# Fused attention and two expert layers: first k and q split on ScalarE and VectorE, idle products ahead of the scores, and the expert embeddings prepared in the first pair

## The reference

```python
# attention: B, H, S, D = 4, 8, 576, 64
scores = q @ k.T / sqrt(D) + cum[:, None] - cum[None, :]   # cum = cumsum(log(clip(f, 1e-4, 1)))
scores = where(causal, -1e9, scores)
x = softmax(scores) @ v                                    # laid out as 2304 tokens of 512
# dense layer: 512 -> 2048 -> 512
h = x @ w_in
g = where(h >= 1, h, where(h <= -1, 0, (h + 1) ** 2 / 4))
x = g @ w_out
# experts: N, D, E, F = 2304, 512, 8, 1024
xn = x / (norm(x) + 1e-6)
en = expert_emb / (norm(expert_emb) + 1e-6)
logits = xn @ en.T / tau
e = argmax(logits)
out = softmax(logits)[e] * (relu(x @ w1[e]) @ w2[e])
```

## Time and profile before

| | |
|---|---|
| three timed runs | 880.87, 882.09, 882.01 us, median 882.01 |
| the profiled execution | 880.4 us |
| its span, first to last instruction | 878.4 us |
| PE busy | 842.3 us, 96% |
| PEld busy | 796.7 us, 91% |
| DVE busy | 410.5 us, 47% |
| ACT busy | 394.8 us, 45% |
| POOL busy | 366.4 us, 42% |
| share of the chain of waits | PE 88%, ACT 5%, DVE 4%, POOL 1%, issue 1% |
| mean granted TensorE clock | 0.999 |

### The profile page before, as it was taken

The page is one execution under the profiler, slowest core; times in us unless marked ns, Lnnn a source line. Parts: engine busy times, 40 slices in busy tenths (PEclk is TensorE's granted clock), DMA queues, the critical chain, the costliest instruction groups (busy, mean ns, idle before and its releaser), DMA issues.

```text
span 878.4 us, 13981 instructions
## 1 busy us (share of the span) xinstructions
PE 842.3 (96%) x5138; PEld 796.7 (91%) x5139; DVE 410.5 (47%) x1001; ACT 394.8 (45%) x906; POOL 366.4 (42%) x370
## 2 busy tenths in 40 slices
PE   4999999999989999999999999999999999999995
PEld 3888888888989999999999999999998998998984
DVE  3777788886555544444444445454425210210201
ACT  4777777776566534434534444343331211211211
POOL 7755787784465411201201020074411492010394
PEclk9999999999999999999999999999999999999999
DMA  5667888872200121031021021432233364213140
GB/s 181 178 205 219 237 256 256 257 251 80 56 1 1 47 80 49 7 102 52 28 99 54 28 100 50 124 132 61 61 109 96 103 172 132 77 44 120 35 138 25
DMA packets 66334, 94.58 MB, mean 108 GB/s; under 512 B 6662, under 2 KB 42502, under 8 KB 66256
## 3 DMA queue, kind: packets, MB, share of 16 engines
q1 hardware_dynamic: 58160, 79.43, 30.0%
q10 hardware_dynamic: 6336, 9.44, 3.0%
q0 software_dynamic: 1760, 4.72, 1.4%
HBM read 69.82 MB, written 24.27 MB: 107 GB/s over the span
## 4 chain that ended last, share of the span: by engine, by line
PE 88%; ACT 5%; DVE 4%; issue 1%; POOL 1%; DMA 0%; SPq 0%; ACTq 0%; POOLq 0%; DVEq 0%
PE psum L1370 23%; PE psum L1372 22%; PE psum L1371 22%; PE psum L1304 6%; PE psum L1345 6%; PE psum L1329 4%; DVE ptl L1000 1%; PE psum L1310 1%; ACT pth L792 1%; ACT xo L798 1%; PE psum L1425 1%; DVE g L1029 1%; ACT pr L783 1%; PE psum L1424 1%; PE psum L1314 1%
## 5 line engine op out<-in xcount | busy, mean ns | idle before, releaser
L1370 PE MATMUL psum<-xh,winh 128*128 128x384 f32 x384 | 130.9, 341 | 3.5 <-ACT hpos L829 3.5
L1371 PE MATMUL psum<-xl,winh 128*128 128x384 f32 x384 | 128.4, 334 | 0.0
L1370 PE MATMUL psum<-gh,wouth 128*128 128x384 f32 x384 | 128.4, 334 | 0.0
L1372 PE MATMUL psum<-xh,winl 128*128 128x384 f32 x384 | 128.3, 334 | 0.0
L1372 PE MATMUL psum<-gh,woutl 128*128 128x384 f32 x384 | 128.3, 334 | 0.0
L1371 PE MATMUL psum<-gl,wouth 128*128 128x384 f32 x384 | 128.3, 334 | 0.0
L829 ACT ACTIVATE hpos<-psum,minus 128x384 f32<-128x384 f32 x96 | 55.8, 581 | 149.8 <-DVE hclip L1026 149.5
L1029 DVE TENSOR_TENSOR g<-hpos,hsq 128x384 f32<-128x384 f32 x96 | 63.3, 660 | 112.9 <-ACT hsq L831 112.9
L783 ACT ACTIVATE pr<-pr,mmin 128x64 f32<-128x64 f32 (+2 forms) x144 | 81.7, 568 | 38.3 <-DVE mmin L984 38.3
L622 POOL TENSOR_TENSOR xst<-xst 128x384 f32<-128x384 f32 x24 | 24.3, 1012 | 178.7 <-DMA xst<-rinv_d 178.7
L1142 DVE SCALAR_TENSOR_TENSOR hl<-psum,hh 128x384 fp32r<-128x384 f32 x48 | 26.7, 557 | 141.0 <-ACT hh L860 141.0
(11 more groups left out here) (216 smaller groups left out, 1938.2 us busy)
## 6 DMA issues: line engine op xcount, KB each, us to landing
praw<-moe_w SPq DMA_DIRECT2D x48, 256.0 KB, 2.7
qraw<-q SPq DMA_DIRECT2D x16, 576.0 KB, 5.5
vraw<-vk SPq DMA_DIRECT2D x16, 320.0 KB, 2.9
xh<-yh_d SPq DMA_DIRECT2D x20, 256.0 KB, 4.1
xl<-yl_d SPq DMA_DIRECT2D x20, 256.0 KB, 4.5
kraw<-k SPq DMA_DIRECT2D x16, 288.0 KB, 4.4
c<-cum_d SPq DMA_DIRECT2D x32, 144.0 KB, 4.1
xa_d<-xo SPq DMA_DIRECT2D x16, 288.0 KB, 3.7
```

The costliest lines, as they stand in the source:

```text
L1370: nc.tensor.matmul(psum_at, ah, bh, start=start, stop=False)
L1371: nc.tensor.matmul(psum_at, ah, bl, start=False, stop=False)
L1372: return nc.tensor.matmul(psum_at, al, bh, start=False, stop=stop)
```

## The change

- **First split.** k and q of pair 0 are copied to their high parts by ScalarE, right behind its logarithm, and their low parts are made by VectorE, right behind cum. POOL starts with the mask copies. Its split of pair 1 waits for `q_l`.
- **Idle products.** 22 products of 512 columns of `ident_b` with itself go ahead of the first score on TensorE, into bank `PY`. Nothing reads them.
- **Embeddings.** They are loaded at the start, into a part of `xo`, which is free until pair 0's results. The squared sum lies between VectorE's two subtractions, the square root behind ScalarE's copies, the refinement and scaling at n = -1, the transposes on TensorE at n = 0, and the split at n = 1 and 2. In the refinement a tensor_scalar with two pointer scalars stands in place of two tensor_tensor instructions. `attend_early` waits for `ent_ok`, since both use bank 6.
- **Transfers.** v of pair 0 goes behind the first two c transfers instead of ahead of cum, and k and q of pair 1 go ahead of c of pair 1.
- The wait of `y_high(0)` for the embeddings becomes one for the stores of the attention.

```diff
+    WARM = 22
...
-        scratch = ysq[0:E].rearrange("e m t -> e (m t)")
-        emb, emb_sq, norm_e = scratch[:, 0:DM], scratch[:, DM:2 * DM], scratch[:, 2 * DM:2 * DM + 3]
...
+        emb, emb_sq, norm_e = xo[0:E, 0, 0, 0:DM], xo[0:E, 0, 1, 0:DM], xo[0:E, 1, 0, 0:3]
...
             load_qk(0)
-            load_v(0)
+            sp.dma_start(emb, expert_emb).then_inc(emb_in, 16)
+            sp.dma_start(tau_sb[:], tau.unsqueeze(0).to_broadcast([P, 1])).then_inc(emb_in, 16)
             sp.wait_ge(cum_ok, 1)
             sp.dma_start(cum_d, fc).then_inc(cum_out, 16)
             sp.wait_ge(cum_out, 16)
             load_c(0)
+            load_v(0)
+            load_qk(1)
             load_c(1)
-            load_qk(1)
             load_v(1)
...
-            sp.dma_start(emb, expert_emb).then_inc(emb_in, 16)
-            sp.dma_start(tau_sb[:], tau.unsqueeze(0).to_broadcast([P, 1])).then_inc(emb_in, 16)
...
             def split_qk(p):
                 par = p % 2
                 pool.wait_ge(k_in, 16 * (p + 1))
+                if p == 1:
+                    pool.wait_ge(q_l, 1)
...
 
-            split_qk(0)
             pool.wait_ge(const_step, 4)
...
+            act.wait_ge(k_in, 16)
+            nc.scalar.copy(kh[:, 0, :], kraw[:]).then_inc(k_h, 1)
+            act.wait_ge(q_in, 16)
+            nc.scalar.copy(qh[:, 0], qraw[:]).then_inc(q_h, 1)
+            act.wait_ge(esq_ok, 1)
+            nc.scalar.activation(norm_e[:, 1:2], norm_e[:, 0:1], ACT.Sqrt).then_inc(eroot_ok, 1)
...
+                if n == 1:
+                    act.wait_ge(en_turned, 1)
+                    nc.scalar.copy(ent[:, :, 0:E], psum[:, RB, 0:KD * E].rearrange(
+                        "p (k e) -> p k e", e=E)).then_inc(ent_h, 1)
...
-                    act.wait_ge(emb_in, 32)
+                    for b in range(2):
+                        act.wait_ge(x_out[b], 32 * (PAIRS // 2))
+                        act.wait_ge(r_out[b], 16 * (PAIRS // 2))
...
-                if u == 4:
-                    act.wait_ge(esq_ok, 1)
-                    nc.scalar.activation(norm_e[:, 1:2], norm_e[:, 0:1], ACT.Sqrt).then_inc(eroot_ok, 1)
-                if u == 13:
-                    act.wait_ge(en_turned, 1)
-                    nc.scalar.copy(ent[:, :, 0:E], psum[:, RB, 0:KD * E].rearrange(
-                        "p (k e) -> p k e", e=E)).then_inc(ent_h, 1)
...
+            dve.wait_ge(k_h, 1)
+            nc.vector.tensor_tensor(kl[:, 0, :], kraw[:], kh[:, 0, :].bitcast(F32), ALU.subtract).then_inc(k_l, 1)
+
+
+            dve.wait_ge(emb_in, 32)
+            nc.vector.tensor_tensor_reduce(out=emb_sq, in0=emb, in1=emb, scale=1.0, scalar=0.0, op0=ALU.mult,
+                                           op1=ALU.add, accum_out=norm_e[:, 0:1]).then_inc(esq_ok, 1)
+            dve.wait_ge(q_h, 1)
+            nc.vector.tensor_tensor(ql[:, 0], qraw[:], qh[:, 0].bitcast(F32), ALU.subtract).then_inc(q_l, 1)
...
+                if n == -1:
+                    step(nc.vector.reciprocal(tau_inv[:], tau_sb[:]))
+                    dve.wait_ge(eroot_ok, 1)
+                    step(nc.vector.tensor_scalar_max(norm_e[:, 1:2], norm_e[:, 1:2], 1.0e-30))
+                    step(nc.vector.reciprocal(norm_e[:, 2:3], norm_e[:, 1:2]))
+                    step(nc.vector.tensor_scalar(norm_e[:, 2:3], norm_e[:, 2:3], norm_e[:, 0:1], norm_e[:, 1:2], ALU.mult,
+                                                 ALU.add))
+                    step(nc.vector.tensor_scalar(norm_e[:, 2:3], norm_e[:, 2:3], 0.5, 1.0e-6, ALU.mult, ALU.add))
+                    step(nc.vector.reciprocal(norm_e[:, 1:2], norm_e[:, 2:3]))
+                    nc.vector.tensor_scalar(emb, emb, norm_e[:, 1:2], None, ALU.mult).then_inc(en_ok, 1)
+                if n == 2:
+                    dve.wait_ge(ent_h, 1)
+                    nc.vector.tensor_tensor(ent[:, :, E:2 * E], psum[:, RB, 0:KD * E].rearrange(
+                        "p (k e) -> p k e", e=E), ent[:, :, 0:E].bitcast(F32), ALU.subtract).then_inc(ent_ok, 1)
...
-                if u in (3, 8, 13):
-                    embeddings(u)
...
             pe.wait_ge(const_ok, 2)
+
+            for n in range(WARM):
+                nc.tensor.matmul(psum[:, PY, :].rearrange("p (a b) -> p a b", a=4), ident_b[:],
+                                 ident_b[:].unsqueeze(1).to_broadcast([P, 4, P]), start=True, stop=True)
...
                 pe.wait_ge(pt_l, FILLS * p + 2)
                 pe.wait_ge(vsplit, p + 1)
+                pe.wait_ge(ent_ok, 1)
                 if p >= 1:
                     pe.wait_ge(x_late_b, p)
...
+                if n == 0:
+                    pe.wait_ge(en_ok, 1)
+                    for m in range(KD):
+                        x = nc.tensor.transpose(psum[:, RB, m * E:(m + 1) * E], emb[:, m * P:(m + 1) * P],
+                                                ident[0:E, 0:E])
+                    x.then_inc(en_turned, 1)
...
-                if u == 12:
-                    pe.wait_ge(en_ok, 1)
-                    for m in range(KD):
-                        x = nc.tensor.transpose(psum[:, RB, m * E:(m + 1) * E], emb[:, m * P:(m + 1) * P],
-                                                ident[0:E, 0:E])
-                    x.then_inc(en_turned, 1)
```

More of the change, by code:

```diff
@@ L955, in _, with step, refine_root @@
         def _(dve):
+            steps = [0]
+            def step(x):
+                steps[0] += 1
+                x.then_inc(dve_step, 1)
+                dve.wait_ge(dve_step, steps[0])
+            def refine_root(root, square, t):
+                step(nc.vector.tensor_scalar_max(root, root, 1.0e-30))
+                step(nc.vector.reciprocal(t, root))
+                step(nc.vector.tensor_tensor(t, t, square, ALU.mult))
+                step(nc.vector.tensor_tensor(t, t, root, ALU.add))
+                step(nc.vector.tensor_scalar(t, t, 0.5, 1.0e-6, ALU.mult, ALU.add))
+                step(nc.vector.reciprocal(root, t))
             nc.vector.memset(fz, 0.0)
@@ L1058, in _ @@
                     hidden(H_EARLY.index(n))
-            steps = [0]
-            def step(x):
-                steps[0] += 1
-                x.then_inc(dve_step, 1)
-                dve.wait_ge(dve_step, steps[0])
-            def refine_root(root, square, t):
-                step(nc.vector.tensor_scalar_max(root, root, 1.0e-30))
-                step(nc.vector.reciprocal(t, root))
-                step(nc.vector.tensor_tensor(t, t, square, ALU.mult))
-                step(nc.vector.tensor_tensor(t, t, root, ALU.add))
-                step(nc.vector.tensor_scalar(t, t, 0.5, 1.0e-6, ALU.mult, ALU.add))
-                step(nc.vector.reciprocal(root, t))
+                if n == -1:
[12 more added lines that the diff above has]
+                        "p (k e) -> p k e", e=E), ent[:, :, 0:E].bitcast(F32), ALU.subtract).then_inc(ent_ok, 1)
             def y_low(c, blocks):
@@ L1120, in choose @@
                 chain(nc.vector.tensor_tensor(pick[:, part, :], zc[:, 2], by_expert(mc[:, 1]), ALU.is_equal))
-            def embeddings(u):
-                if u == 3:
-                    dve.wait_ge(emb_in, 32)
-                    nc.vector.tensor_tensor_reduce(out=emb_sq, in0=emb, in1=emb, scale=1.0, scalar=0.0,
-                                                   op0=ALU.mult, op1=ALU.add, accum_out=norm_e[:, 0:1]).then_inc(
-                                                       esq_ok, 1)
-                elif u == 8:
-                    step(nc.vector.reciprocal(tau_inv[:], tau_sb[:]))
-                    dve.wait_ge(eroot_ok, 1)
-                    refine_root(norm_e[:, 1:2], norm_e[:, 0:1], norm_e[:, 2:3])
-                    nc.vector.tensor_scalar(emb, emb, norm_e[:, 1:2], None, ALU.mult).then_inc(en_ok, 1)
-                else:
-                    dve.wait_ge(ent_h, 1)
-                    nc.vector.tensor_tensor(ent[:, :, E:2 * E], psum[:, RB, 0:KD * E].rearrange(
-                        "p (k e) -> p k e", e=E), ent[:, :, 0:E].bitcast(F32), ALU.subtract).then_inc(ent_ok, 1)
             def relu_low(at, f_, high, to):
```

## The result

Four timed runs of the changed kernel took 875.8 to 876.4 us, median 876.1; four of before beside them 880.9 to 882.1, median 881.5. The ratio is 0.9939, 95% interval 0.9927 to 0.9952. A second series, made with the experiments, gave 875.8 against 881.1, ratio 0.9937 (0.9925 to 0.9950). The change saves 5.4 us, 0.6%. The traced execution of after took 876.39 (span 874.2), against 880.4 (878.4) of before: 4.0 less.

What follows compares the result with a forecast made beforehand. TensorE's chain bounds the kernel, with losses at the POOL-bound start, the slow first products and two dense-layer waits. Dense layer 3.9 plus start 1.3 gives 5.2 us off the 881.3 mean: 876.1, own range 873.9 to 879.4, 8-in-10 range 873.9 to 880.3.

Steps and rivals of the forecast that it cites:

- The dense layer, 3.9: Dense layer: taking the square root, small instructions, transposes and last copy out saves 3.9 us; 2.7 to 4.1 possible.
- the second gap: Dense layer, TensorE's 1.95 us wait for hpos before 263.54, behind VectorE's eight small instructions: costs 2.11 us.
- The start, 1.3: First two pairs: last exponential of pair 0 and POOL's ql for pair 1 come earlier, saving 1.3 us; bounds 0 and 2.8.
- the first mask: Pair 0's start: it needs c, whose second transfer lands at 11.6, so it starts at about 11.8 us.
- the last exponential of pair 0: End of pair 0: summed durations put it at 21.45 us against 22.79, 1.3 earlier; called the weakest part.
- v of pair 0 is issued at 9.0 and lands after 3.0: Pair 1's split on POOL: v lands at 12.0, so ql of pair 1 is ready at 20.15, 1.6 us earlier.
- ql of pair 1 later than 21 us: Sign of being wrong about v's landing time; the forecast had ql of pair 1 ready at 20.15 us.
- products of 448 columns at 0.57 after 12 us: Sign on TensorE in the start that its clock is at half rate, against the forecast.
- Clock falls once: Rival, chance 0.08: TensorE's clock falls again before pair 1, losing 3.1 us; total gain 2.1, time 879.2.
- Held steps: Rival, chance 0.22: POOL holds VectorE's embedding tensor_scalar steps in the start, which loses 0.85 us or more; time 879.8.
- More than the sum: Rival, chance 0.08: POOL is not late and the ring keeps its slack; start gives 2.8, total 6.7, time 874.6.
- Slower: Rival, chance 0.06: TensorE stays at 1.2 GHz through pairs 0 and 1, costing 8.6 us against 3.9; time 886.0.

Runs made afterwards that it cites:

- Kernel 10: Before, with the refinement's two one-element tensor_tensor instructions replaced by one tensor_scalar, embeddings still in the dense layer; median 878.2 us, ratio 0.9967.
- kernel 9: Before, with idle products (3 and 8) filling TensorE's two gaps in the dense layer; median 880.6 us, ratio 0.9993.
- Kernel 4: After, with v of pair 0 issued before the wait for cum, k and q of pair 1 behind the first c; median 876.1 us, ratio 0.9935.
- kernel 7: Kernel 4 with the embedding steps ahead of VectorE's first mask and 14 idle products ahead of pair 1; median 875.0 us, ratio 0.9933.
- kernel 2: After, with the embeddings back in the dense layer, so the start's part alone; median 883.4 us, ratio 1.0022.
- 8: Kernel 7 with ql of pair 1 made by VectorE instead of POOL, and 4 idle products ahead of pair 1; median 875.4 us, ratio 0.9937.
- 6: Kernel 2 with 22 more idle products between pair 0's last score and pair 1's first; median 881.6 us, ratio 0.9996.
- kernel 1: Before, with only the embeddings' work moved into the first pair, start otherwise as before; median 879.2 us, ratio 0.9969.
- kernel 3: After, without the 22 idle products at the start; median 876.7 us, ratio 0.9944.

## Why the prediction was right in sum and wrong in one term

**The dense layer, 3.9: right in a quiet run, one in which the clock doesn't fall there, and short in the timed ones.** The rest shrank by 4.0 in every trace with the embeddings gone (834.3 to 834.6 in eight traces). Kernel 10 bears out the second gap as a term of its own: forecast 2.11 with both slow instructions in it, measured 1.9 for these two. What the term lacked is the clock. The prediction argued that 1.95 us of standing leave TensorE at full rate; that rested on one trace, and two of the four with that gap show the opposite. In such a run the dense layer costs 1.6 more, and the change takes that away too. By the traces a quiet run of before takes 39.8 + 838.5 + 2.0 around the span = 880.3, and one with the fall 881.9; the timed medians of 881.1 to 881.7 lie between. The timed runs have no traces, but each lists its mean granted clock, 0.999 in the first trace of before and 0.996 in the second. Of the fifty of before, fifteen list 0.999 and took 880.3 to 881.1 (median 880.8); twenty-eight list 0.995 or 0.996 and took 881.0 to 883.9 (median 882.0). So it is likely that more than half of the runs have a fall. It is not all of the spread: seven took over 882.7, more than the slowest of the fifteen and one fall of 1.6 give. A late tau, as in kernel 9's trace, is one candidate; what those runs lost, no trace shows. The narrower spread of after (875.7 to 876.6 in nine runs) goes with both.

**The start, 1.3: failed.** Four traces with the start of before (before twice, kernels 9 and 10) have the turn at 39.54 to 39.94, mean 39.76; after has it at 39.73 and 39.92. By kernel 10 the timed runs agree: it took 878.2 and after 875.8, 2.4 apart, and their rests differ by 2.2. By the fifteen runs of before at 0.999 they leave more room: their median, 880.8, is 4.8 above the 876.0 of all nine runs of after, of which the dense layer explains 4.0, and the two traced executions of after (876.4 and 876.6) were the slowest of their series. So the start gave nothing in the traces, and in a typical run something between 0.2 and 0.8 that is not placed.

By its steps: the first score (forecast 11.2, measured 9.88), ql of pair 0 (9.3, 8.93), the first mask (11.6 to 11.8, 11.48) and the last exponential of pair 0 (21.45, 20.98) came as early as forecast or earlier. The step that failed is "v of pair 0 is issued at 9.0 and lands after 3.0, and ql of pair 1 is ready at 20.15". It took the landing time from a trace in which fewer transfers ran at once. v came 0.9 later than forecast; q, whose landing the step left out, held POOL for another 0.97; and ql ended at 22.08, 1.9 late. Kernel 4 bears this out: with v issued first, ql ends at 19.99 and the turn comes 1.3 earlier. The lower bound of the term, 0 "if v lands 1.3 us later", was the case in its amount, by v and q together.

**Why the total was right all the same.** The forecast took 5.2 from the mean of four runs, 881.3, which is 0.9 above the traced execution. That 0.9 was not a constant of the kernel but most likely the dense layer's clock in part of the runs (the fifty took 881.6 in the mean, the fifteen at 0.999 took 880.8), and the change removed it. So up to 1.3 too much for the start met 0.9 and 0.1 too little for the dense layer. That the two errors nearly cancelled was luck. From the traced time alone with the start at nothing, 880.4 - 4.0 = 876.4 is what the traced execution of after took.

**The rivals.** Two of the prediction's own signs of being wrong came: ql of pair 1 later than 21 us, and products of 448 columns at 0.57 after 12 us. *Clock falls once* came true as a mechanism, in both traces of after, but not with its price: it stretches a pair 0 that waits for ql anyway. Its price shows where ql is early: from kernel 4 to kernel 7, in whose trace the clock doesn't fall, the turn comes 0.9 earlier and the median is 1.1 lower. Kernel 7 changes two things for it, the place of the steps and the idle products, and they were not tried apart. The Trainium skill, "TensorE: Matmul & The Clock Gate", Why this matters for your kernels, warns of gaps over some 3 us; here the clock fell behind gaps of 0.92, 1.34, 1.46, 1.79 and, in two of four traces, 1.95, so by these rows the rule is no assurance for shorter ones. The 5.28 of kernel 2, in which it fell, agrees with it. *Held steps* is refuted for the one-element instructions (0.14 to 0.26 throughout, beside a working POOL in kernels 7 and 10) and true for the scaling of 512 columns, 0.47 free against 0.58 to 1.38. POOL did not work from 12.0 on, as the rival had it, but from 12.93, since v was late. *More than the sum*: kernel 4 removed POOL's lateness and the median stayed; the slack of ScalarE and VectorE's ring that it counts on went, by kernels 7 and 8, to the half rate at least in part. *Slower* did not happen, but the start alone is slower by 0.22%, by its mechanism: TensorE at half rate between waits.

**The parts do not add up.** The embeddings alone save 2.5 us, the start alone costs 1.8, both together save 5.4. Each alone has its own disorder in the first two pairs: with the embedding steps on top of POOL's late start TensorE is at half rate up to 23.7, and the fast start leaves it standing for 5.28. Together, as I read it, the one fills the other's wait. That the embedding steps keep the fast start from losing its clock ahead of pair 1 is read from kernels 2 and 6 against after; that this is all of the difference was not tested.

## What to carry to other kernels

Trace the kernel before twice. One trace shows one outcome of the clock behind each gap, and the distance between a traced time and the median of the timed runs is a question, not a constant to carry over. A gap on TensorE is worth its length plus, in part of the runs, what the half rate behind it costs, 1.6 us here. Look at the small instructions too: one tensor_scalar in place of two tensor_tensor of one element gave 2.9 of the 5.4. And before a start is made faster, find the last transfer that the next stage waits for: what comes earlier in front of it only becomes a wait.

## What the runs showed of the hardware

- The clock fell behind gaps of 0.9 to 2 us, and not each time: the same gap of 1.95 us in the same kernel left it at 1.00 once and took it to a granted 0.57 (264 to 268) once, and the 2.42 of after ahead of pair 1 left it at full rate (64 columns in 0.27). A stretch at half rate behind one lasted 3.2 to 6.7 us.
- The granted clock does not show the first slow stretch. In kernel 1 it reads 1.00 from 12 to 23.7, where products of 448 columns take 0.57; behind a gap the same durations go with 0.50. It does count the end of the span, where TensorE has nothing left to do (0.53 from 876 to 878.4 in the first trace of before).
- When the clock first rises varies: 7.3 us after the first product in the first trace of before, 6.6 in the second, 10.9 in kernel 1, some 11.4 in kernel 3.
- Two tensor_tensor of one element on VectorE took 0.98 and 1.22 beside a working POOL, a tensor_scalar with both operands as pointers 0.26 (kernel 10). The holding goes both ways: POOL's tensor_scalar of v, 0.72 elsewhere, took 1.69 in kernel 4 beside VectorE's ql.
- q of pair 1 (576 KB) landed 6.9 us after its issue with the transfers at 363 GB/s (12 to 14 us of after); the median over the kernel is 5.4.
